# Attention with hashed masks, then two expert layers: the way from the last token sum to the first sorted tile

## The reference

```python
def _moe2_ref(x, expert_emb, tau, w1, w2):          # x: 1536 x 512, E = 8, F = 1024
    xn = x / (norm(x) + 1e-06)
    en = expert_emb / (norm(expert_emb) + 1e-06)
    logits = xn @ en.T / tau
    expert_idx = argmax(logits, axis=1)
    probs = exp(logits - logits.max(-1)); probs /= probs.sum(-1) + 1e-09
    gate_w = probs[arange(N), expert_idx]
    for e in range(E):
        mask = expert_idx == e
        out[mask] = gate_w[mask, None] * (relu(x[mask] @ w1[e]) @ w2[e])
```

## Time and profile before

| what | us |
|---|---|
| median of three timed executions | 1612.83 |
| the profiled execution | 1612.79 |
| its span, first to last instruction | 1611.1 |
| TensorE busy in the span | 1578.6 (98%) |
| VectorE busy | 682.7 (42%) |
| ScalarE busy | 507.7 (32%) |
| GpSimd busy | 311.4 (19%) |
| TensorE's share of the chain that ended last | 90% |

### The profile page before, as it was taken

One profiled execution on the slowest core, in us unless ns is written; L12 is line 12 of the kernel. 1 busy time (PEld: TensorE's weight loads), 2 busy tenths in 40 slices (PEclk: granted clock), 3 DMA queues, 4 the chain that ended last, 5 costly groups with the idle time before them and its releaser, 6 DMA issues.

```text
span 1611.1 us, 21916 instructions
## 1 busy us (share of the span) xinstructions
PE 1578.6 (98%) x7637; PEld 1318.6 (82%) x7638; DVE 682.7 (42%) x1237; ACT 507.7 (32%) x933; POOL 311.4 (19%) x522
## 2 busy tenths in 40 slices
PE   7999999999999999999999999999999999899997
PEld 6999998778888888888888888888888887778886
DVE  5888788351211211322221121122232255787666
ACT  4777777211100101211210111021121133476554
POOL 4455443200210120030030021003003000132222
PEclk8999999999999999999999999999999999799999
DMA  6554554100110110110020011011002121574310
GB/s 153 136 128 112 126 121 146 71 1 0 52 53 1 52 52 0 52 52 0 0 100 4 0 52 52 0 52 52 0 0 105 40 79 72 187 291 148 140 46 25
DMA packets 45592, 110.96 MB, mean 69 GB/s; under 512 B 5926, under 2 KB 7974, under 8 KB 45552
## 3 DMA queue, kind: packets, MB, share of 16 engines
q1 hardware_dynamic: 41248, 100.52, 20.1%
q0 software_dynamic: 3504, 8.14, 1.5%
q10 hardware_dynamic: 800, 1.77, 0.5%
HBM read 81.57 MB, written 8.39 MB: 56 GB/s over the span
## 4 chain that ended last, share of the span: by engine, by line
PE 90%; DVE 3%; issue 2%; POOL 2%; DMA 2%; ACT 1%; POOLq 0%; DVEq 0%; ACTq 0%
PE psum L444 25%; PE psum L446 25%; PE psum L445 25%; PE psum L682 3%; PE psum L671 2%; PE psum L695 2%; PE psum L696 1%; PE psum L672 1%; PE psum L653 1%; DVE row_min L1263 1%; PE psum L707 1%; PE psum L971 1%; DVE pt_lo L1253 1%; PE psum L799 1%; DMA x_row<-x_rows,idx_now 1%
## 5 line engine op out<-in xcount | busy, mean ns | idle before, releaser
L1123 ACT ACTIVATE h_hi<-psum 128x512 fp32r<-128x512 f32 x192 | 115.0, 599 | 890.5 <-PE psum L446 890.5
L444 PE MATMUL psum<-xt_lo,w_hi 128*128 128x512 f32 x768 | 305.5, 398 | 0.2 <-DVE xt_lo L1356 0.2
L446 PE MATMUL psum<-xt_hi,w_lo 128*128 128x512 f32 x768 | 304.5, 396 | 0.0
L445 PE MATMUL psum<-xt_hi,w_hi 128*128 128x512 f32 x768 | 304.4, 396 | 0.0
L444 PE MATMUL psum<-w_lo,h_hi 128*128 128x512 f32 x768 | 302.3, 394 | 0.0
L446 PE MATMUL psum<-w_hi,h_lo 128*128 128x512 f32 x768 | 299.3, 390 | 0.0
L445 PE MATMUL psum<-w_hi,h_hi 128*128 128x512 f32 x768 | 299.1, 389 | 0.0
L1514 DVE SCALAR_TENSOR_TENSOR h_lo<-psum,h_hi 128x512 fp32r<-128x512 f32 x192 | 132.8, 692 | 368.5 <-ACT h_hi L1123 368.5
L1569 DVE SCALAR_TENSOR_TENSOR tok<-psum,route,tok 128x512 f32<-128x512 f32 x84 | 57.5, 745 | 355.3 <-PE psum L446 355.3
L477 POOL CAST w_hi<-w_raw 128x512 fp32r<-128x512 f32 x64 | 40.0, 626 | 823.1 <-PE psum L446 813.8
L444 PEld LDWEIGHTS psum<-xt_lo,w_hi 128*128 128x128 f32 x768 | 144.6, 188 | 35.1 <-DVE xt_lo L1356 0.4
(11 more groups left out here) (264 smaller groups left out, 2026.8 us busy)
## 6 DMA issues: line engine op xcount, KB each, us to landing
w_raw<-in_moe_w_dram SPq DMA_DIRECT2D x25, 2048.0 KB, 8.2
w_raw_odd<-in_moe_w_dram SPq DMA_DIRECT2D x4, 2048.0 KB
k_hh<-k_hi SPq DMA_DIRECT2D x32, 192.0 KB, 3.0
w_raw_even<-in_moe_w_dram SPq DMA_DIRECT2D x3, 2048.0 KB
x_rows<-tok SPq DMA_DIRECT2D x14, 256.0 KB, 2.4
k_raw<-in_k_dram SPq DMA_DIRECT2D x8, 384.0 KB, 3.0
v_raw<-in_v_dram SPq DMA_DIRECT2D x16, 192.0 KB, 3.4
k_b<-k_lo SPq DMA_DIRECT2D x16, 192.0 KB, 3.4
```

The costliest lines, as they stand in the source:

```text
L444: pe.matmul(acc, a[0], b[1], start=start, stop=False)
L445: pe.matmul(acc, a[0], b[0], start=False, stop=False)
L446: return pe.matmul(acc, a[1], b[0], start=False, stop=stop)
L1123: act.activation(h_s[0][:, f, :], psum[:, f % 4, :], ACT.Relu).then_inc(m1.h_hi, 1)
```

## The change

It changes the order and the place of the steps between the last token sum and tile 0, in these parts.

- The sum of tile 11 is done in two halves of 256 columns, and so are its turn (PSUM banks 0 and 7) and ScalarE's copy (`turn_half`, `last_token`).
- Of the eight products of gathered rows and `diag` (four blocks, two matmuls each), those of the first two blocks stay ahead of the last logits. Those of the other two go behind the table part of tile 10, ahead of the last rows of tile 11 (`gathered_rows`).
- TensorE reads the first tile's numbers out of the table one step earlier (`f == 4`). VectorE's fourth piece of `w1_lo` (block 3) moves from behind the sum of tile 10 and the cell of tile 9, ahead of a table sum (`add_part`), to behind the choice of tile 10, ahead of the sum of tile 11.
- The softmax weights are made on GpSimd, except for the three reciprocals, which stay on VectorE, and the Exp and square root on ScalarE. The sum over 8 experts becomes three additions (4, 2 and 1 columns). It stands in GpSimd's program between the gather of tile 0 and that of tile 1.
- ScalarE and VectorE read the bound of the first expert's tiles (`first_end`) before Exp and before the last reciprocal, and run the first expert's tiles ahead of the loop over experts, which TensorE does already.

```diff
@@ gpsimd, behind the gather of tile 0
+        pool.wait_ge(s_total_in, 1)
+        pool.tensor_tensor(g1[:], logit[:], row_bc(4), ALU.subtract).then_inc(s_p_step, 1)
+        pool.wait_ge(s_norm, 1)
+        pool.tensor_tensor(inv, inv, squares, ALU.mult).then_inc(s_p_step, 1)
+        pool.wait_ge(s_p_step, 2)
+        pool.tensor_tensor(inv, inv, per_tok[:, 2, :], ALU.add).then_inc(s_p_step, 1)
+        pool.wait_ge(s_p_step, 3)
+        pool.tensor_scalar(inv, inv, 0.5, 1e-6, ALU.mult, ALU.add).then_inc(s_p_step, 1)
+        pool.wait_ge(s_norm, 2)
+        pool.tensor_tensor(g1[:], g1[:], row_bc(3), ALU.mult).then_inc(s_act_in, 1)
+        pool.wait_ge(s_act_out, 4)
+        for n in (4, 2):
+            pool.tensor_tensor(g1[:, :, 0:n], g1[:, :, 0:n], g1[:, :, n:2 * n], ALU.add).then_inc(s_p_step, 1)
+            pool.wait_ge(s_p_step, 4 + 4 // n)
+        pool.tensor_tensor(squares, g1[:, :, 0], g1[:, :, 1], ALU.add).then_inc(s_p_step, 1)
+        pool.wait_ge(s_p_step, 7)
+        pool.tensor_scalar(per_tok[:, 1, :], squares, 1e-9, None, ALU.add).then_inc(s_p_sum, 1)
         pool.wait_ge(m2.routed, 1)
@@ tensor
-            if t == HOT and f == 5:
+            if t == HOT and f == 4:
@@
-        turn_token(TT - 1, 0)
-        pe.wait_ge(s_diag, 1)
-        pe.wait_ge(s_xrow, 16)
+        pe.wait_ge(s_squares, TT - 1)
+        pe.wait_ge(s_tok_half, 1)
+        turn_half(0, 0).then_inc(s_turn_half, 1)
+        pe.wait_ge(m1.y, E * TT + 1)
+        turn_half(1, 7).then_inc(s_turned, 1)
+        gathered_rows((0, 1))
         for kd in range(KD):
-            pe.matmul(psum[:, 2 + kd, 0:P], x_row[:, kd * P:(kd + 1) * P], diag[:], start=True, stop=False)
-        token_logits(TT - 1, 1)
+            if kd % 2 == 0:
+                pe.wait_ge(s_copied, TT + kd // 2)
+            mm = pe.matmul(psum[:, 1, 0:E], x_t[:, kd, :], emb_t[:, kd, :], start=(kd == 0), stop=(kd == KD - 1))
+        mm.then_inc(s_logits, 1)
         last_rows(HOT)
         ...
         table_part(HOT, 0)
+        gathered_rows((2, 3))
         last_rows(TT - 1)
@@ scalar
-                    token(2 * CT + 3, 0)
+                    last_token()
@@
         first_x_hi()
+        act.wait_ge(s_start, 1)
+        first_end = act.value_load(start_i[0:1, 1:2], min_val=1, max_val=SLOTS)
         act.wait_ge(s_act_in, 4)
         act.activation(g1[:], g1[:], ACT.Exp).then_inc(s_act_out, 1)
-        act.wait_ge(s_start, 1)
         act.wait_ge(s_x_lo, 1)
+        tiles2(0, 0, 0, first_end)
@@ vector, find_cell
             if t == TT - 1:
+                dve.wait_ge(s_act_out, 3)
+                dve.reciprocal(per_tok[:, 3, :], per_tok[:, 2, :]).then_inc(s_norm, 1)
                 dve.wait_ge(s_total, 1)
@@ vector, last expert
                         choose(2 * CT - 1 + i, 1)
+                        if i == CT - 1:
+                            w1_lo2(0, w1_raw, (KD - 1,))
@@
+                    if last and tile == TT - 1:
+                        for half, done in ((slice(0, 256), s_tok_half), (slice(256, 512), m1.y)):
+                            dve.scalar_tensor_tensor(tok[:, tile, half], psum[:, 4 + i, half], route[:, e, tile:tile + 1],
+                                                     tok[:, tile, half], ALU.mult, ALU.add).then_inc(done, 1)
+                        find_cell(HOT, 6)
+                        continue
@@
-                        if i < CT - 1:
+                        if i < CT - 2:
                             w1_lo2(0, w1_raw, (i + 1,))
@@ vector, behind the last find_cell
-        dve.wait_ge(s_act_out, 3)
-        ...
-        link(dve.reciprocal(inv, root))
-        link(dve.tensor_tensor(inv, inv, per_tok[:, 0, :], ALU.mult))
-        link(dve.tensor_tensor(inv, inv, root, ALU.add))
-        link(dve.tensor_scalar(inv, inv, 0.5, 1e-6, ALU.mult, ALU.add))
-        link(dve.reciprocal(inv, inv))
-        link(dve.tensor_tensor(g1[:], logit[:], row_bc(4), ALU.subtract))
-        link(dve.tensor_tensor(g1[:], g1[:], row_bc(3), ALU.mult))
-        dve.sem_inc(s_act_in, 1)
+        inv = per_tok[:, 3, :]
+        dve.wait_ge(s_p_step, 4)
+        dve.reciprocal(inv, inv).then_inc(s_norm, 1)
         dve.wait_ge(s_begin, 1)
@@
         dve.sem_inc(m2.routed, 1)
-        dve.wait_ge(s_act_out, 4)
-        link(dve.tensor_reduce(per_tok[:, 0, :], g1[:], AX.X, ALU.add))
-        link(dve.tensor_scalar(per_tok[:, 1, :], per_tok[:, 0, :], 1e-9, None, ALU.add))
+        first_end = dve.value_load(start_i[0:1, 1:2], min_val=1, max_val=SLOTS)
+        dve.wait_ge(s_p_sum, 1)
         link(dve.reciprocal(per_tok[:, 2, :], per_tok[:, 1, :]))
         dve.sem_inc(s_p_ready, 1)
```

More of the change, by code:

```diff
@@ L611, in _, with row_bc @@
         gather(x_row[:], x_rows, first_idx[:], s_xrow)
+        squares, inv = per_tok[:, 0, :], per_tok[:, 3, :]
+        def row_bc(i):
+            return per_tok[:, i, :].unsqueeze(2).to_broadcast([P, TT, E])
+        pool.wait_ge(s_total_in, 1)
[15 more added lines that the diff above has]
+        pool.tensor_scalar(per_tok[:, 1, :], squares, 1e-9, None, ALU.add).then_inc(s_p_sum, 1)
         pool.wait_ge(m2.routed, 1)
@@ L838, in last_rows @@
                 mm = pe.matmul(psum[:, 2 + kd, 0:P], tok[:, t, kd * P:(kd + 1) * P], hot[:, t - HOT, :],
-                               start=False, stop=t == TT - 1)
+                               start=t == HOT and kd >= 2, stop=t == TT - 1)
             if t == TT - 1:
@@ L934, in _, with gathered_rows, turn_half @@
         expert(E - 1, last=True)
-        turn_token(TT - 1, 0)
-        pe.wait_ge(s_diag, 1)
-        pe.wait_ge(s_xrow, 16)
+        def gathered_rows(kds):
+            pe.wait_ge(s_diag, 1)
+            pe.wait_ge(s_xrow, 16)
+            for kd in kds:
+                pe.matmul(psum[:, 2 + kd, 0:P], x_row[:, kd * P:(kd + 1) * P], diag[:], start=kd < 2, stop=False)
+        def turn_half(half, bank):
+            for kd in (2 * half, 2 * half + 1):
+                a = kd % 2 * P
+                tr = pe.transpose(psum[:, bank, a:a + P], tok[:, TT - 1, kd * P:kd * P + P], ident[:])
+            return tr
+        pe.wait_ge(s_squares, TT - 1)
[4 more added lines that the diff above has]
+        gathered_rows((0, 1))
         for kd in range(KD):
-            pe.matmul(psum[:, 2 + kd, 0:P], x_row[:, kd * P:(kd + 1) * P], diag[:], start=True, stop=False)
-        token_logits(TT - 1, 1)
+            if kd % 2 == 0:
+                pe.wait_ge(s_copied, TT + kd // 2)
+            mm = pe.matmul(psum[:, 1, 0:E], x_t[:, kd, :], emb_t[:, kd, :], start=(kd == 0), stop=(kd == KD - 1))
+        mm.then_inc(s_logits, 1)
         last_rows(HOT)
@@ L1094, in token, with last_token @@
                            accum_out=per_tok[:, 0, t:t + 1]).then_inc(s_squares, 1)
+        def last_token():
+            t = TT - 1
+            act.wait_ge(s_logits, t)
+            act.wait_ge(s_turn_half, 1)
+            act.copy(x_t[:, 0:2, :].rearrange("p k i -> p (k i)"), psum[:, 0, 0:256]).then_inc(s_copied, 1)
+            act.wait_ge(s_turned, TT)
+            act.copy(x_t[:, 2:4, :].rearrange("p k i -> p (k i)"), psum[:, 7, 0:256]).then_inc(s_copied, 1)
+            act.wait_ge(s_copied, TT + 1)
+            act.activation(psum[:, 0, :], tok[:, t, :], ACT.Square,
+                           accum_out=per_tok[:, 0, t:t + 1]).then_inc(s_squares, 1)
         def copy_gate(m, c, bank):
@@ L1175, in y_tile, with tiles2 @@
             act.activation(y_row[:], psum[:, 4, :], ACT.Copy, scale=p_now[:, 0:1]).then_inc(s_y2, 1)
-        def expert2(e, u, more=True):
-            first, end = tile_range(act, e)
+        def tiles2(e, u, first, end, more=True):
             with act.Fori(first, end) as i:
@@ L1195, in _ @@
         first_x_hi()
+        act.wait_ge(s_start, 1)
+        first_end = act.value_load(start_i[0:1, 1:2], min_val=1, max_val=SLOTS)
         act.wait_ge(s_act_in, 4)
         act.activation(g1[:], g1[:], ACT.Exp).then_inc(s_act_out, 1)
-        act.wait_ge(s_start, 1)
         act.wait_ge(s_x_lo, 1)
+        tiles2(0, 0, 0, first_end)
         with act.Fori(0, E // 2 - 1) as e2:
-            for u in range(2):
-                expert2(2 * e2 + u, u)
-        expert2(E - 2, 0)
-        expert2(E - 1, 1, more=False)
+            for u in (1, 0):
+                e = 2 * e2 + 2 - u
+                tiles2(e, u, *tile_range(act, e))
+        tiles2(E - 1, 1, *tile_range(act, E - 1), more=False)
         every = act.value_load(start_i[0:1, E:E + 1], min_val=E, max_val=SLOTS)
@@ L1571, in expert @@
                     if last and c == CH - 1:
-                        find_cell(2 * CT - 1 + i, 6 if i == CT - 1 else 2)
-                        if i < CT - 1:
+                        find_cell(2 * CT - 1 + i, 2)
+                        if i < CT - 2:
                             w1_lo2(0, w1_raw, (i + 1,))
@@ L1652, in g_lo, with tiles2 @@
                               ALU.subtract).then_inc(s_g_lo, 1)
-        def expert2(e, u, more=True):
```

(11 more changed lines are left out.)

3 lines of the change are left out of this document (2 added, 1 removed).

## The result

The changed kernel takes 1616.05 us (median of 22 runs, 1614.04 to 1618.33), the kernel before beside it 1612.37 us (22 runs): the ratio is 1.0017, with a 95% interval of 1.0010 to 1.0025. So it became slower by 2.7 us by the ratio (1.6 to 4.0 by the interval) and by 3.7 by the medians, where the prediction had it faster by 2.5 and its range ended at 1612.9. The profiled execution took 1616.55 us, with a span of 1614.9, 3.8 more than before.

The account below looks back on a forecast made before the run. Bound: TensorE's way to tile 0 and the softmax weights' way through DMAs. The smaller gain, the weights' 2.55 - 0.17 = 2.4 us, from 1612.8 gave 1610.4, stated as 1610.3 us; range 1607.3 to 1612.9.

Parts of the forecast that it names:

- the two runners: TensorE to tile 0 (gain 3.15 + 0.3 us) and softmax weights through the DMAs (2.4 us); the smaller gain counts.
- The sign that I named for the second: In tile 2, ScalarE waits longer than 1.86 us for the weights if the forecast is right.
- Up to H: Stretch to the last one-hot matrix: last choice starts at 1377.1 instead of 1379.66, 2.55 us sooner.
- H: End of the last `hot`, the last one-hot matrix: 1382.35 before, forecast at 1379.8.
- Half clock: From the last choice into tile 0, TensorE's clock assumed at half: tile 0 starts 3.15 us sooner, at 1385.3.
- the rival of the full clock: Clock may not fall before tile 0: TensorE gains 6.0 us, 1606.8 if the long gather also shortens; chance 0.13.
- the 0.6 us won behind H: Between H and the begin column at half clock: TensorE late, column at H+3.25 instead of H+3.86; 1.2 us at full clock.
- From H to the weights: GpSimd's steps, Exp and reciprocal after H: weights at H+8.15 instead of H+7.98, so 2.4 us sooner overall.
- The rival of a slow GpSimd: GpSimd's four last softmax steps take 0.635 us each, weights come 1.3 us later: 1611.6; chance 0.17.
- The gather of tile 1's row costs nothing: This gather queues on GpSimd behind the softmax sum; TensorE turns the row 8 us into tile 0: cost zero.
- landings are taken as now: The two gathers on the weights' way land as before, though weight loads move; bounds 3.65 and 8.12 us.
- Gathers behind a weight load: One more weight load ahead of a gather costs 4.5 us: 1614.8, slower than before; chance 0.08.

Follow-up runs that it names:

- 55 increments: Changed kernel with 55 harmless semaphore increments added to GpSimd's program at an idle place: 1608.22 us, ratio 0.9979.
- 24 increments: Changed kernel with 24 harmless semaphore increments added at the same idle place of GpSimd's program: 1608.24 us, ratio 0.9962.
- the base of the same length: Kernel before with 64 harmless semaphore increments added to GpSimd's program at its idle place: 1611.91 us, ratio 0.9991.
- the kernel with the softmax back: Changed kernel with the softmax weights computed on VectorE again, no increments: 1609.03 us, ratio 0.9983.
- 12 increments: Changed kernel with 12 harmless semaphore increments added at the same idle place of GpSimd's program: 1609.24 us, ratio 0.9977.

## Why the prediction was wrong, step by step

*The bound.* TensorE's way to tile 0 and the weights' way through the DMAs are the two runners, as said. The sign that I named for the second, ScalarE's longer wait for the weights, came by luck: 8.59 us in tile 1 is the stall's. With 55 increments it waits 1.00 us in tile 1 and 1.73 in tile 2, and TensorE 0.36 in tile 2 where it waited 0.33 before: there the two runners gain alike, and not 2.4 against 3.45.

*Up to H.* Right in every piece, and in the sum. Of all that follows, 0.5 us is the lead that this execution has at the copy. The index came at 1369.04, 2.1 us sooner and so 1.6 behind the copy (1.6 said); the rank wait is gone; the moved piece ended at 1372.64 and the sum waited for TensorE, not for it, so it was covered; VectorE started the last choice as soon as it was free (1376.46, with 0.34 us of waiting; 1377.1 said). H is at 1379.08 where I said 1379.8: 3.3 us sooner, 2.8 behind the copy, 2.55 said.

*Half clock.* Wrong, and this is the first failing step: behind the copy tile 0 came 4.2 us sooner, not 3.15, 0.2 of it at H and the rest behind it. The clock stayed full from 1374 to about 1384.4, so the rival of the full clock had the first half of the way right. Its second half failed, since the clock fell all the same, 0.6 us into tile 0 and 1.1 us behind 1.80 us of waiting for the slots, for 3.4 us. But the price was wrong too, not only the choice between two clocks. With 24 increments TensorE runs the same program, and there its clock did fall, near 1377.7 (PEclk is the third number from the end):

```profile
1377.00:1378.00 1.00, 0.69 (x5) 0.58 (x4) 0.76 (x5) 0.00 (x0) 0.21 (x1) 0.83 1.00 358
1378.00:1380.00 2.00, 2.00 (x12) 1.70 (x10) 1.40 (x7) 0.58 (x1) 0.66 (x3) 0.50 1.03 390
```

```profile
1379.87 0.15 DVE L1675 COPY begin_col<-psum 96x1 f32<-96x1 f32 x1 [0.20 <-PE psum L995]
```

VectorE reached the begin column at H+2.56 there and waited 0.20 us for TensorE, where I had TensorE late until H+3.25. The four row products (0.67 us) were done before `hot` was, so that the last rows began 0.1 us behind H. Tile 0 came 16.5 us behind the copy, against 16.35 at full clock and 20.55 before. The term that fails is the 0.6 us won behind H: 1.3 to 1.5 were won at either clock.

*From H to the weights.* VectorE spent 2.28 us from H to the begin column (1381.36), where I said 3.25. The price of GpSimd's steps was taken well: 0.20 to 0.30 us for the small ones, 0.35 and 0.38 for 96 columns (0.3 and 0.45 said), ready at H+7.5 (H+8.15 said). VectorE waited 1.81 us for the sum and not at all for the norm part, and the table load stood behind the register load, as said. The weights came 3.3 us sooner behind the copy (2.4 said). The rival of a slow GpSimd falls. Nor does a wait for the shared port show in these steps: none took longer than 0.38 us. I said that VectorE's stream would begin at H+8.3, and it began at H+7.8.

*"The gather of tile 1's row costs nothing", "landings are taken as now".* The first held for TensorE, which did not wait for the 3.94 us, but not for the way of the weights: GpSimd's idle time ahead of its copy of the indices (3.16 us) now ends with this landing, and the scatter and the gather of the weights stand behind it. GpSimd had ended its last register step at 1389.95 and the row landed at 1390.69, so 0.7 us of that landing is on the chain, where I had nothing. The second did not: the gather of tile 1's weights took 7.23 us, where the one on the chain before took 5.99 (that was tile 2's). By itself that is the small part of the error.

*The missing term.* The sum fails at the step in which I put nine more instructions on GpSimd and priced their run time alone. An instruction also shifts all behind it in the program, and the next piece of the program was now wanted between the last register step and the scatter. Its price is the difference between the changed kernel and the same with 55 increments: 6 us by the ratios, 7.8 by the medians, 8.8 behind the copy. Without it the change gives 1608.2, inside the range and 2.1 below the forecast; against the base of the same length that is 3.7 us by the medians, 4.7 behind the copy and 1.9 by the ratios, where 2.5 was predicted. No rival had this mechanism. *Gathers behind a weight load* gave 1614.8 and is nearest by its number, but not by its cause: it had the load delay the gathers themselves; the runs show that the load alone makes no gap (the kernel with the softmax back, and the one with 55 increments), and that what it delays to harm is a fetch of GpSimd's program.

What of the trace of before could have warned me: the page's table of queues lists instruction packets, and the view of the DMA queues between 1405 and 1406 shows one (it starts at 1405.85, 8.6 us behind the start of the scatter and inside GpSimd's 6.89 us of idle time for its gathered row):

```profile
q14 instruction: 1, 0.01, 1.9%
```

With 64 increments it is gone from there and one stands at 1241.79 instead. So the kernel before fetches too, but in a wait, and pays nothing for it. That the packet is GpSimd's, and nine instructions away from the scatter, could not be read from that trace; that an added instruction on GpSimd can move it out of the wait could.

## What to carry to other kernels

Before an edit that adds instructions to an engine is judged, its trace belongs searched for idle time that ends with "issue" and has a packet of an instruction queue in it; a loss there has nothing to do with the edit's own work, and shifting the program by a few dozen harmless instructions at an idle place shows it within one run. Compare a change and its base with the same shift, or a border will be taken for the change: here it turned a gain of 3 us into a loss of 3. And an engine that issues small transfers on the path should pass such a border while the queues are quiet.

## What the runs showed of the hardware

- A fetch of GpSimd's program in the middle of its work: a gap of 2.50 us with empty queues, 4.96 and 4.70 us with a 2 MB weight load under way, each time at the same place of the program, where 0.83 us pass without a fetch. In all three the scatter starts 2.0 us after the instruction packet (1394.48 and 1396.47, 1397.74 and 1399.76, 1393.81 and 1395.77); what the load adds is the time until the packet is served: about 3.0 and 2.7 us instead of 0.5.
- The rule of where the fetch is asked for stays open. With 12 increments it came at 1392.0, with 24 at 1368.0, with 55 near 1242.6; the last two times differ by more than 31 instructions of work, since GpSimd stands in a wait between them. The Trainium skill, "Advanced Engine Details and Errata", section "ISA Cache", gives lines of 16 KB, 256 instructions, and only two of them; in this trace the packets of queue 14, that of GpSimd's extra fetch among them, are 8 KB (15 packets, 0.12 MB in the table of queues), and only those of queue 8 are 16 KB (24 packets, 0.39 MB).
- Preparing a scatter or gather took GpSimd 1.04 us at 1386.75, and 1.96 and 1.92 us at 1396.47 and 1398.74, while VectorE ran its 128x1024 differences without a pause from 1395.17 to 1399.8; the next, at 1400.96 with VectorE idle, took 0.95 again. Nine of the ten that began under such differences ahead of 1412 in the kernels with and without increments took 1.82 to 1.99 us. The durations fit a wait for one VectorE instruction (1.2 us each), but no run here took VectorE's stream away, and in the changed kernel's trace a scatter at 1436.81 took 2.28 us beside 128x512 ones, where one at 1396.43 with the softmax back took 0.95 us although a 128x1024 one began under it. So the cause is argued and not shown. The Trainium skill, "SBUF — State Buffer", section "SBUF: two separate sides", has an operation with two inputs in SBUF hold the shared port only against a GpSimd operation that reads SBUF; whether preparing a gather is one, no run here shows.
- TensorE's clock stayed full through waits of 0.92 us and less between 1374 and 1380 in the changed kernel, and fell in the kernel before, with waits of 0.92 us and less as well. The waits' lengths alone don't tell the two apart. Nor does TensorE's program: with 24 increments it is that of the changed kernel, with waits of 0.92 and 0.30 us at the same places, and the clock fell near 1377.7, 4.9 us sooner behind the copy.
